# First search first: a smaller first k load, q of tile 0 in two halves, and constants made early, in a fused attention and expert kernel

## The chip, the cores and the metric

The kernel runs on one NeuronCore of a Trainium2 chip. The core has TensorE (PE, matmuls and their weight loads, PEld), VectorE (DVE), ScalarE (ACT), GpSimd (POOL) and SyncE (SP, which here issues nearly all DMAs). Each engine works through its own queue in order, and the engines wait for one another only by semaphores. The metric is the device time of one execution, in microseconds (us); lower is better.

## The reference

Attention with a top-k mask, then a top-1 mixture of eight experts, then a dense layer pair with a rational activation:

```python
B, H, S, D = 2, 8, 576, 64          # q, k, v
scores = (q @ k.T) / sqrt(D)
kth = partition(scores, -32)[..., -32:-31]      # the 32nd largest of each row
attn = softmax(where(scores >= kth, scores, -1e9))
x = (attn @ v) as [1152, 512] rows
# experts: argmax gate, capacity 288, relu(x @ w1[e]) @ w2[e], times the gate's weight
# dense: h = x @ w_in; g = (a0 + a1 h + a2 h^2 + a3 h^3) / (1 + |b0||h| + |b1| h^2 + 1e-6); g @ w_out
```

## The kernel before

**Tiling.** The 1152 rows of the two batches form NT = 9 tiles of 128 queries. With H = 8 heads this gives NH = 72 units of one tile and one head, numbered `i` with `n, h = divmod(i, H)`. Tile 4 is mixed, half of it from each batch. Each unit's scores are 128 x 576. In fp32r precision one number is a high part, made by a copy to fp32r on ACT, and a low part, the difference, made by DVE or POOL; k and q are split so, and then turned (transposed) by PE into PSUM and copied out by ACT.

**The search.** DVE finds the 32nd largest of each row of 576 scores. `greater(x)` takes the larger of each pair (288 numbers) from PSUM and the copy in SBUF, POOL's `sum_pairs(x)` and `less_greater(x)` make the lesser ones (both plain 128x288 operations). Then DVE takes steps: `M1` to `M4` (MAX8, the next eight largest), `R1` to `R3` between them (MATCH_REPLACE8, strikes these eight out), `L1`, `LR`, `L2` the same for the lesser ones, and `JOIN` and `FIN` that give the limit. `R1` waits for `less_greater`. Two units are interwoven: loop step `i` of DVE does the first half of unit `i`, the second half of unit `i-1`, and `greater(i+2)`.

**The slots.** Outside DVE, every engine has a function `slot(i)` that is called for each unit in order. PE: `scores(i+2)`, `times_v(i-3)`, then the scores' turns of unit `i-2` (`turn_scores`, `less_max`, `drop`), then `k_turn` and `q_turn`. ACT: `short_of(i-2)`, `scores_out(i+2)` (PSUM to SBUF), `x_out`, `k_high`, `q_high`, `exps(i-2)`, then `k_out` and `q_out` of what PE turned. POOL: `max_parts(i-1)`, `less_greater(i+1)`, `sums`, `k_low`, `sum_pairs(i+2)`, `q_low`. `k_pieces(i)`, `k_heads(i)` and `q_pieces(i)` say which head of k and which part of q is due in a slot; the table `USE` numbers all uses of the PSUM banks for turns in order. `scores(x)` waits for `greater(x-1)`, as both use the same PSUM tile.

**The beginning.** Ahead of the slots stands an order written out by hand. SP issues k of heads 0 and 1, q of tile 0, k of heads 2 to 7, v of batch 0, then waits until the first q is split (`s_ql`), and issues q of tile 1, k of batch 1, the gate weights, the coefficients and v of batch 1. PE begins with nine `fill` matmuls on a tile of ones (L1707), which compute nothing that is used, then turns k of head 0, q high and q low of heads 0 to 3, and k of head 1; `scores(0)`, fills, `scores(1)`, turns of k of head 2, q of heads 4 to 7, k of head 3. ACT (the lines that matter are these):

```python
k_high(0)
q_high(0)
k_high(1)
k_out(0, 0); k_out(0, 1); q_out(0, 1, 0)
k_out(1, 0); k_out(1, 1)
k_high(2)
scores_out(0)
k_high(3)
scores_out(1)
```

DVE does `k_low(0)`, the low part of q, `k_low(1)`, the copy of turned q high (L874), `greater(0)`, `greater(1)`, and then its loop, which begins with `M1` of unit 0. POOL splits heads 2 and 3, does `sum_pairs(0)`, `sum_pairs(1)`, `less_greater(0)`, then sets constants (L756, ones beside v; L757, zeros; `tri` and others from L759), then the slots.

**Later.** After the last unit PE, DVE and ACT compute the gate and the slots of the tokens, and then PE runs the experts and the dense layers (L1757 to L1759, three products for each fp32r pair). Weight loads are issued by SP as buffers come free.

## Time and profile before

| | |
|---|---|
| median of 3 runs | 777.88 us (777.29 to 779.7) |
| the profiled execution | 775.52 us |
| its span (first to last instruction) | 773.7 us |
| PE busy | 745.3 us (96%) |
| DVE busy | 663.3 us (86%) |
| ACT busy | 499.9 us (65%) |
| POOL busy | 383.2 us (50%) |

The profile is one execution on the chip. Its timeline gives for each instruction start, duration, engine, source line, operation, output <- input and, in brackets, the idle time of that engine before it and what ended it. "SPq" is the queue of SP, whose duration is that of issuing. `pairs` are the halves that the search works on, `best` the eights that it found, `scores` the copies in SBUF, `bank` any PSUM tile, `k_split` the high and low parts of k. The granted TensorE clock is full in all forty slices of the page.

### The profile page before, as it was taken

What the parts mean: (1) busy time and instruction counts of PE and PEld (TensorE: products, weight loads), DVE (VectorE), ACT (ScalarE), POOL (GpSimd) and SP (SyncE); (2) the same over time, 40 slices, a digit from 0 to 9 for tenths busy, and PEclk for the clock granted to TensorE, in tenths of its full rate; (3) what the DMA queues carried; (4) which work ended last, traced back from release to release, by engine and by line L of the source; (5) the groups of instructions that cost most, each with busy time, mean ns of one, the idle gap of its engine ahead of it and who ended that gap; (6) DMA issues with size and microseconds to landing.
All of it is one profiled execution on the core that took longest, in us unless ns stands there. A gap on an engine that the chain in (4) does not pass through costs nothing.

```text
span 773.7 us, 15880 instructions
## 1 busy us (share of the span) xinstructions
PE 745.3 (96%) x5503; PEld 697.7 (90%) x5503; DVE 663.3 (86%) x1682; ACT 499.9 (65%) x911; POOL 383.2 (50%) x550
## 2 busy tenths in 40 slices
PE   7899999999999989899999999999999999999998
PEld 5788899898888888799999999999998998999996
DVE  3999999999999999986767666767679999988885
ACT  6677777656667776466454444445578878777674
POOL 4746665545457786446000000000369879666764
PEclk9999999999999999999999999999999999999999
DMA  9840000800000303004657675769740002001001
GB/s 188 196 150 14 2 16 1 215 19 16 14 3 15 110 2 110 2 1 161 221 166 236 179 262 164 242 175 258 168 149 28 1 1 82 1 0 40 3 1 41
DMA packets 59853, 70.63 MB, mean 91 GB/s; under 512 B 21858, under 2 KB 39522, under 8 KB 59780
## 3 DMA queue, kind: packets, MB, share of 16 engines
q1 hardware_dynamic: 58340, 64.98, 29.5%
q0 software_dynamic: 1440, 4.72, 1.8%
q8 instruction: 41, 0.67, 0.4%
q14 instruction: 32, 0.26, 0.1%
HBM read 55.53 MB, written 14.16 MB: 90 GB/s over the span
## 4 chain that ended last, share of the span: by engine, by line
PE 54%; DVE 30%; issue 7%; POOL 4%; ACT 3%; DMA 1%; DVEq 0%; SPq 0%; POOLq 0%; ACTq 0%
PE bank L1757 14%; PE bank L1758 14%; PE bank L1759 14%; DVE best L900 9%; DVE pairs L902 6%; PE bank L1617 3%; DVE best L921 3%; DVE pairs L883 3%; DVE pairs L919 3%; DVE r L1206 2%; PE bank L1593 2%; PE bank L1583 2%; DMA k_rows<-in_k 1%; PE bank L1677 1%; DVE joined L930 1%
## 5 line engine op out<-in xcount | busy, mean ns | idle before, releaser
L1206 DVE RECIPROCAL r<-c 128x384 f32<-128x384 f32 x48 | 122.4, 2550 | 16.5 <-POOL c L836 15.9
L1279 ACT ACTIVATE probsT<-bank 96x768 f32<-96x768 f32 x72 | 58.1, 807 | 90.6 <-PE bank L1600 88.2
L900 DVE MAX8 best<-pairs 128x8 f32<-128x288 f32 x288 | 115.3, 440 | 0.0
L1617 PE MATMUL bank<-v_rows,probsT 96*128 96x65 f32 (+1 forms) x960 | 105.7, 263 | 2.6 <-ACT probsT L1279 2.3
L1617 PEld LDWEIGHTS bank<-v_rows,probsT 96*128 96x128 f32 (+1 forms) x960 | 102.0, 181 | 6.8 <-ACT probsT L1279 5.6
L902 DVE MATCH_REPLACE8 pairs<-best,pairs 128x288 f32<-128x288 f32 x216 | 94.1, 440 | 0.0
L806 POOL DMA_INDIRECT x_rows_of_others<-slots_out,slot_index_of_others x3 | 4.4, 1477 | 180.5 <-DMA slots_out<-y_blocks 179.8
L1420 ACT ACTIVATE hTh<-bank 128x288 fp32r<-128x288 f32 x64 | 26.3, 411 | 102.5 <-PE bank L1759 100.6
L698 POOL TENSOR_TENSOR pairs<-scores 128x288 int32<-128x288 int32 x72 | 57.6, 800 | 65.7 <-ACT scores L1265 65.4
L1088 DVE TENSOR_TENSOR wl<-raw,wh 128x1024 fp32r<-128x1024 f32 x60 | 72.9, 1217 | 17.2 <-ACT wh L1387 17.2
L1757 PE MATMUL bank<-xTh,wh 128*128 128x288 f32 x256 | 75.7, 296 | 1.0 <-issue 0.7
L1759 PE MATMUL bank<-hTh,wl 128*128 128x288 f32 x256 | 76.1, 297 | 0.0
L1758 PE MATMUL bank<-hTl,wh 128*128 128x288 f32 x256 | 75.8, 296 | 0.0
L1757 PE MATMUL bank<-hTh,wh 128*128 128x288 f32 x256 | 75.7, 296 | 0.0
L1758 PE MATMUL bank<-xTl,wh 128*128 128x288 f32 x256 | 75.6, 295 | 0.0
L1759 PE MATMUL bank<-xTh,wl 128*128 128x288 f32 x256 | 75.1, 293 | 0.0
L836 POOL TENSOR_TENSOR c<-c,h 128x384 f32<-128x384 f32 x48 | 48.6, 1013 | 40.1 <-ACT h L1503 40.0
L1757 PE MATMUL bank<-x2h,wh 128*128 128x384 f32 x192 | 65.4, 341 | 0.0
L1759 PE MATMUL bank<-x2h,wl 128*128 128x384 f32 x192 | 64.7, 337 | 0.0
L1758 PE MATMUL bank<-x2l,wh 128*128 128x384 f32 x192 | 64.5, 336 | 0.0
L921 DVE MAX8 best<-pairs 128x8 f32<-128x288 f32 x144 | 64.5, 448 | 0.0
L1387 ACT ACTIVATE wh<-raw 128x1024 fp32r<-128x1024 f32 x60 | 62.9, 1051 | 0.0
(188 smaller groups left out, 2234.3 us busy)
## 6 DMA issues: line engine op xcount, KB each, us to landing
raw<-in_moe_w SPq DMA_DIRECT2D x15, 2048.0 KB, 9.0
slots_in<-zeros SPq DMA_DIRECT2D x18, 256.0 KB
raw<-in_moe_w_in SPq DMA_DIRECT2D x8, 512.0 KB
slot_rows<-slots_in SPq DMA_DIRECT2D x28, 144.0 KB, 8.8
slots_out<-y_blocks SPq DMA_DIRECT2D x28, 144.0 KB, 8.1
v_rows<-in_v SPq DMA_DIRECT2D x16, 144.0 KB, 4.7
out_rows<-out_rows SPq DMA_DIRECT2D x9, 256.0 KB, 2.0
q_rows<-in_q SPq DMA_DIRECT2D x8, 256.0 KB, 3.1
```

Of the source, the lines that this page charges most:

```text
L698: nc.gpsimd.tensor_tensor(pr[x % NPR][:, 1].bitcast(I32), of[:, 0:HS], of[:, HS:S], ALU.add).then_inc(s_ps, 1)
L900: ins = nc.vector.max(best, cur)
L902: ins = nc.vector.match_replace(cur, best, cur, NEG)
L921: ins = nc.vector.max(best, cur)
L1088: nc.vector.tensor_tensor(piece(wl[slot], c), piece(raw[which], c), piece(wh[slot], c).bitcast(F32), ALU.subtract).then_inc(s_wl, 1)
L1206: nc.vector.reciprocal(rS[x][:], cS[x][:]).then_inc(s_d2, 1)
L1279: nc.scalar.activation(pT[x % 2][:], turned(x)[0:KP, 0:KJ * P], ACT.Exp, scale=SCALE).then_inc(s_ex, 1)
L1387: nc.scalar.activation(piece(wh[slot], c), piece(raw[which], c), ACT.Copy).then_inc(s_wh, 1)
L1617: last = nc.tensor.matmul(dst[r_, :], pT[x % 2][:, j * P + r_.start:j * P + r_.stop], vn[:, bb * H + h, j, :], start=(j == 0), stop=(j == ...
L1757: nc.tensor.matmul(dst, ah, bh, start=start, stop=False)
L1758: nc.tensor.matmul(dst, ah, bl, start=False, stop=False)
L1759: return nc.tensor.matmul(dst, al, bh, start=False, stop=stop)
```

## The change

- **Loads.** k of head 0, first half of q of tile 0 (heads 0 to 3), k of head 1, second half of q, k of heads 2 and 3, k of heads 4 to 7: six loads where there were three. The second half of q has a semaphore of its own. SP waits for `s_ql` of 2 (both halves split) ahead of q of tile 1; all later waits on `s_ql` and `s_qh` count one higher (shown once below).
- **First q.** ACT makes the high part in two halves; DVE makes the low part of the first half, POOL of the second.
- **Order.** ACT copies `scores_out(0)` ahead of `k_out(1)` and `k_high(2)`. DVE does `M1` of unit 0 and `k_low(2)` between `greater(0)` and `greater(1)`, then `R1` and `L1` of unit 0. `k_low(1)` comes behind the copy of turned q. PE's fills are 2, 2 and 3 in place of 2 and 5, and the turns of head 1 come behind `scores(0)`.
- **Constants.** POOL makes the ones beside v, the zeros, `tri` and the small ones ahead of its first `sum_pairs`. `k_low(2)` goes to DVE.
- **Tile 0.** Heads 3 to 7 of k are turned in slots 0 to 4 (before: 4 to 7 in slots 0 to 3), the second q half in slots 0 (high) and 1 (low), and q of tile 1 in slots 4 and 5 in place of 3 and 4. In slots 0 to 6 ACT does `k_high` and `scores_out` first and the copies of turned k and q ahead of `exps`; PE turns k and q ahead of the scores' turns; POOL does `k_low` first in slots 2 to 6.

```diff
@@ -383,7 +384,7 @@
-        FIRST_K, FIRST_Q = 4, 2
+        FIRST_K, FIRST_Q = 3, 2
@@ -401,10 +402,14 @@
             n, h = divmod(i, H)
+            if i in (0, 1):
+                return [(0, i, 1)]
             if h == 0:
...
                 return []
+            if n == 0:
+                return {4: [(1, 0, 0)], 5: [(1, 1, 0)], 7: [(1, 0, 1)]}.get(h, [])
             return {3: [(n + 1, 0, 0)], 4: [(n + 1, 1, 0)], 7: [(n + 1, 0, 1)]}.get(h, [])
@@ -426,7 +431,7 @@
         for what in (("k", 0, 0), ("k", 0, 1), ("q", 0, 0, 0), ("q", 0, 1, 0), ("k", 1, 0), ("k", 1, 1),
-                     ("k", 2, 0), ("k", 2, 1), ("q", 0, 0, 1), ("q", 0, 1, 1), ("k", 3, 0), ("k", 3, 1)):
+                     ("k", 2, 0), ("k", 2, 1)):
             next_use(*what)
@@ -466,11 +471,12 @@
         M1, R1, M2, R2, M3, R3, M4, L1, LR, L2, JOIN, FIN = range(12)
-        TK = {}
+        TK = {(0, M1): 1, (0, R1): 2, (0, L1): 3}
         for i in range(NH + 1):
...
                           (i - 1, JOIN), (i, L2), (i - 1, FIN)):
-                if 0 <= x < NH:
+                if 0 <= x < NH and (x, st) not in TK:
                     TK[x, st] = len(TK) + 1
@@ -542,6 +548,12 @@
+            def load_first_q(half, done):
+                c_ = slice(half * (H // 2), (half + 1) * (H // 2))
+                sp.dma_start(qn[:].rearrange("p (h d) -> p h d", h=H)[:, c_, :],
+                             q[0, c_, 0:P, :].rearrange("h s d -> s h d")).then_inc(done, 16)
             def load_k(i, lo, hi):
@@ -549,14 +561,17 @@
-            load_k(0, 0, 2)
-            load_q(0)
-            load_k(1, 2, H)
+            load_k(0, 0, 1)
+            load_first_q(0, s_q)
+            load_k(4, 1, 2)
+            load_first_q(1, s_qb)
+            load_k(1, 2, 4)
+            load_k(2, 4, H)
             load_v(0, 0, 2)
             load_v(1, 2, H)
-            sp.wait_ge(s_ql, 1)
+            sp.wait_ge(s_ql, 2)
             load_q(1)
-            load_k(2, H, 2 * H)
+            load_k(3, H, 2 * H)
             for c in range(DC):
@@ -564,7 +579,7 @@
-            sp.wait_ge(s_ql, 2)
+            sp.wait_ge(s_ql, 3)
             load_q(2)
@@ -675,7 +690,7 @@
             def q_low(n):
-                pool.wait_ge(s_qh, n + 1)
+                pool.wait_ge(s_qh, n + 2)
                 pool.wait_ge(s_pf, filled("q", n - 1, 1, 1))
@@ -728,14 +743,18 @@
                 n, h = divmod(i, H)
+                if 1 < i < H - 1:
+                    for g in k_heads(i):
+                        k_low(g)
                 if 0 <= i - 1 < NH:
...
                     sums(n - 1)
-                for g in k_heads(i):
-                    k_low(g)
+                if not 1 < i < H - 1:
+                    for g in k_heads(i):
+                        k_low(g)
                 if i + 2 < NH:
@@ -749,23 +768,26 @@
                 nc.gpsimd.memset(t[:, TOPK + LESSER:], -NEG).then_inc(s_inf, 1)
-            for g in (2, 3):
-                k_low(g)
-                sum_pairs(g - 2)
-            less_greater(0)
             nc.gpsimd.memset(vn[:, :, :, D:DV], 1.0).then_inc(s_vo, 1)
             nc.gpsimd.memset(zeros[:], 0.0).then_inc(s_zm, 1)
-            k_low(FIRST_K)
             nc.gpsimd.affine_select(out=tri[:], in_=ones[:].bitcast(F32), compare_op=ALU.is_gt, fill=0.0, base=0,
...
             nc.gpsimd.memset(ohz[:, 0:E].bitcast(F32), 0.0).then_inc(s_sum0, 1)
+            sum_pairs(0)
+            less_greater(0)
+            k_low(FIRST_K)
+            sum_pairs(1)
+            pool.wait_ge(s_qh, 2)
+            pool.wait_ge(s_ql, 1)
+            nc.gpsimd.tensor_tensor(ql[:, DM // 2:], qn[:, DM // 2:], qh[:, DM // 2:].bitcast(F32), ALU.subtract
+                                    ).then_inc(s_ql, 1)
             for i in range((MIXED - 1) * H):
...
             for bb in range(B):
-                pool.wait_ge(s_kl[1], 2 * H - 2)
+                pool.wait_ge(s_kl[1], 2 * H - 3)
                 other = slice((1 - bb) * HALF, (2 - bb) * HALF)
@@ -867,13 +889,14 @@
             dve.wait_ge(s_qh, 1)
-            nc.vector.tensor_tensor(ql[:], qn[:], qh[:].bitcast(F32), ALU.subtract).then_inc(s_ql, 1)
-            k_low(1)
+            nc.vector.tensor_tensor(ql[:, 0:DM // 2], qn[:, 0:DM // 2], qh[:, 0:DM // 2].bitcast(F32), ALU.subtract
+                                    ).then_inc(s_ql, 1)
             dve.wait_ge(s_pf, filled("q", 0, 0, 0))
...
             ins.then_inc(s_pd, 1)
+            k_low(1)
@@ -944,16 +967,23 @@
             greater(0)
+            of_greater(0, M1)
+            k_low(2)
             greater(1)
+            of_greater(0, R1)
+            of_lesser(0, L1)
             for i in range(NH + 1):
                 n, h = divmod(i, H)
-                of_greater(i, M1)
+                if i:
+                    of_greater(i, M1)
                 of_greater(i - 1, M3)
...
                     sums(n - 1)
-                of_greater(i, R1)
+                if i:
+                    of_greater(i, R1)
                 of_greater(i - 1, R3)
-                of_lesser(i, L1)
+                if i:
+                    of_lesser(i, L1)
                 of_greater(i, M2)
@@ -1246,17 +1276,21 @@
             def k_high(g):
-                act.wait_ge(s_k[0 if g < 2 else 1 if g < H else 2], 16)
+                act.wait_ge(s_k[0 if g == 0 else 4 if g == 1 else 1 if g < 4 else 2 if g < H else 3], 16)
                 if g >= KRING:
...
                 act.wait_ge(s_q, 16 * (n + 1 + (n >= MIXED)))
-                if n:
-                    act.wait_ge(s_ql, n)
-                    act.wait_ge(s_pf, filled("q", n - 1, 0, 1))
+                act.wait_ge(s_ql, n + 1)
+                act.wait_ge(s_pf, filled("q", n - 1, 0, 1))
                 nc.scalar.activation(qh[:], qn[:], ACT.Copy).then_inc(s_qh, 1)
+            def first_q_high(half):
+                act.wait_ge((s_q, s_qb)[half], 16)
+                c_ = slice(half * (DM // 2), (half + 1) * (DM // 2))
+                nc.scalar.activation(qh[:, c_], qn[:, c_], ACT.Copy).then_inc(s_qh, 1)
@@ -1300,14 +1334,23 @@
                 n, h = divmod(i, H)
+                if i < H - 1:
+                    for g in k_heads(i):
+                        k_high(g)
+                if i + 2 < NH:
+                    scores_out(i + 2)
                 if 0 <= i - 2 < NH:
                     short_of(i - 2)
-                if i + 2 < NH:
-                    scores_out(i + 2)
+                if i < H - 1:
+                    for k_ in k_pieces(i):
+                        k_out(*k_)
+                    for q_ in q_pieces(i):
+                        q_out(*q_)
                 if i >= 3 and (i - 3) % XG == XG - 1 and i - 3 < LAST * H:
                     x_out((i - 3) // XG)
-                for g in k_heads(i):
-                    k_high(g)
+                if i >= H - 1:
+                    for g in k_heads(i):
+                        k_high(g)
                 if h == 1 and n < LAST:
@@ -1316,34 +1359,31 @@
                     exps(i - 2)
-                for k_ in k_pieces(i):
-                    k_out(*k_)
-                for q_ in q_pieces(i):
-                    q_out(*q_)
+                if i >= H - 1:
+                    for k_ in k_pieces(i):
+                        k_out(*k_)
+                    for q_ in q_pieces(i):
+                        q_out(*q_)
                 if x_piece(i) is not None:
...
             k_high(0)
-            q_high(0)
-            k_high(1)
+            first_q_high(0)
             k_out(0, 0)
...
             q_out(0, 1, 0)
+            k_high(1)
+            scores_out(0)
             k_out(1, 0)
...
             k_high(2)
-            scores_out(0)
-            k_high(3)
+            first_q_high(1)
+            k_high(FIRST_K)
             scores_out(1)
...
             k_out(2, 1)
-            q_out(0, 0, 1)
-            q_out(0, 1, 1)
-            k_high(FIRST_K)
-            k_out(3, 0)
-            k_out(3, 1)
             def gated(t):
@@ -1541,7 +1581,7 @@
                 use = USE["q", n, low, half]
-                pe.wait_ge((s_qh, s_ql)[low], n + 1)
+                pe.wait_ge((s_qh, s_ql)[low], n + 2 if n else half + 1)
                 part = (qh, ql)[low][:].bitcast(F32)
@@ -1686,14 +1726,20 @@
                     times_v(i - 3)
+                if i < H - 1:
+                    for k_ in k_pieces(i):
+                        k_turn(*k_)
+                    for q_ in q_pieces(i):
+                        q_turn(*q_)
                 if 0 <= i - 2 < NH:
...
                     drop(i - 2)
-                for k_ in k_pieces(i):
-                    k_turn(*k_)
-                for q_ in q_pieces(i):
-                    q_turn(*q_)
+                if i >= H - 1:
+                    for k_ in k_pieces(i):
+                        k_turn(*k_)
+                    for q_ in q_pieces(i):
+                        q_turn(*q_)
                 if x_piece(i) is not None:
@@ -1713,18 +1759,15 @@
             q_turn(0, 1, 0)
+            fill(2)
+            scores(0)
+            fill(2)
             k_turn(1, 0)
             k_turn(1, 1)
-            fill(2)
-            scores(0)
-            fill(5)
+            fill(3)
             scores(1)
...
             k_turn(2, 1)
-            q_turn(0, 0, 1)
-            q_turn(0, 1, 1)
-            k_turn(3, 0)
-            k_turn(3, 1)
             pe.wait_ge(s_vo, 1)
```

## Rows read from the trace of the kernel before

**Rows 1.** DVE's waits, 0 to 340 us: waiter <- releaser: us, times, longest.
```profile
DVE pairs L883 <- ACT scores L1265: 5.8, 4, 3.7
DVE k_split L865 <- ACT k_split L1252: 4.7, 1, 4.7
DVE pairs L902 <- POOL pairs L705: 1.1, 2, 0.9
```

**Rows 2.** The chain that ended last, around 319 us: start, us, what.
```profile
319.14 0.44 DVE pairs L883
...
319.71 0.37 PE bank L1571
```

**Rows 3.** Timeline, 0 to 20 us (columns as told above).
```profile
1.06 4.04 PE L1707 MATMUL bank<-ones 128*128 128x512 f32 x9 [1.06 <-POOL ones L663]
...
4.66 0.56 DVE L865 TENSOR_TENSOR k_split<-k_rows,k_split 96x384 fp32r<-96x384 f32 x1 [4.66 <-ACT k_split L1252]
...
4.97 0.63 ACT L1259 ACTIVATE q_rows_high<-q_rows 128x512 fp32r<-128x512 f32 x1 [0.34 <-DMA q_rows<-in_q]
...
5.37 0.69 PE L1536 MATMUL bank<-ident,k_split 96*128 96x96 f32 x6 [0.27 <-DVE k_split L865]
...
6.38 0.63 PE L1549 MATMUL bank<-ident,q_rows_low 128*64 128x128 f32 x4
...
7.04 1.20 ACT L1243 ACTIVATE qT_low<-bank 64x512 fp32r<-64x512 f32 x2 [0.44 <-PE bank L1549]
...
8.38 0.37 PE L1571 MATMUL bank<-kT,qT_high 128*128 128x288 f32 x1 [0.33 <-ACT qT_low L1243]
...
8.86 0.29 PE L1572 MATMUL bank<-kT,qT_low 128*128 128x288 f32 x1
...
10.68 0.52 ACT L1252 ACTIVATE k_split<-k_rows 96x384 fp32r<-96x384 f32 x1 [1.70 <-DMA k_rows<-in_k]
...
11.10 0.63 ACT L1265 ACTIVATE scores<-bank 128x576 f32<-128x576 f32 x1
...
11.76 0.46 DVE L883 TENSOR_TENSOR pairs<-bank,scores 128x288 f32<-128x288 f32 x1 [3.68 <-ACT scores L1265]
...
13.85 0.46 DVE L883 TENSOR_TENSOR pairs<-bank,scores 128x288 f32<-128x288 f32 x1 [1.63 <-ACT scores L1265]
...
14.23 0.45 DVE L900 MAX8 best<-pairs 128x8 f32<-128x288 f32 x1
...
15.61 0.09 DVE L902 MATCH_VALUE_LOAD pairs<-best,pairs 128x8 f32 x1 [0.94 <-POOL pairs L705]
...
18.41 0.46 DVE L883 TENSOR_TENSOR pairs<-bank,scores 128x288 f32<-128x288 f32 x1 [0.34 <-ACT scores L1265]
...
19.75 0.09 DVE L902 MATCH_VALUE_LOAD pairs<-best,pairs 128x8 f32 x1 [0.15 <-POOL pairs L705]
```

**Rows 4.** Groups by line, 0 to 26 us: busy, mean ns | idle before.
```profile
L674 POOL TENSOR_TENSOR k_split<-k_rows,k_split 96x384 fp32r<-96x384 f32 x6 | 6.0, 996 | 9.9 <-ACT k_split L1252 9.8
...
L1222 ACT ACTIVATE kT<-bank 128x288 fp32r<-128x288 f32 x12 | 4.2, 401 | 0.1
...
L705 POOL TENSOR_TENSOR pairs<-pairs 128x288 int32<-128x288 int32 x4 | 3.2, 798 | 0.0
```

**Rows 5.** Issues of the page: count, KB each, us from issue to landing.
```profile
k_rows<-in_k SPq DMA_DIRECT2D x1, 864.0 KB, 8.9
```

**Rows 6.** Tile q_rows, 0 to 60 us: landing of its three loads.
```profile
DMA to landing us min/median/max: 3.2/3.7/5.6
```

**Rows 7.** Timeline, 35 to 42 us: ACT's `scores_out(6)`, `greater(6)`, PE's `scores(7)`, `scores(8)`.
```profile
35.57 0.63 ACT L1265 ACTIVATE scores<-bank 128x576 f32<-128x576 f32 x1
...
36.24 0.45 DVE L883 TENSOR_TENSOR pairs<-bank,scores 128x288 f32<-128x288 f32 x1
...
37.32 0.38 PE L1571 MATMUL bank<-kT,qT_high 128*128 128x288 f32 x1
...
41.24 0.37 PE L1571 MATMUL bank<-kT,qT_high 128*128 128x288 f32 x1
```

More of the change, by code:

```diff
@@ L218, in fused @@
         ys = nc.dram_tensor("slots_out", (SLOTS + 1, DM), F32, kind="Internal").ap()
-        s_k = [sem(f"k_in{i}") for i in range(3)]
+        s_k = [sem(f"k_in{i}") for i in range(5)]
         s_q = sem("q_in")
+        s_qb = sem("first_q_second_half_in")
         s_v = [sem(f"v_in{i}") for i in range(3)]
@@ L574, in _ @@
             for n in range(3, MIXED + 2):
-                sp.wait_ge(s_ql, n)
+                sp.wait_ge(s_ql, n + 1)
                 load_q(n)
@@ L601, in _ @@
             for n in range(MIXED + 2, NT):
-                sp.wait_ge(s_ql, n)
+                sp.wait_ge(s_ql, n + 1)
                 load_q(n)
@@ L1528, in k_turn @@
                 use = USE["k", g, half]
-                if g < 2:
+                if g < 3:
                     pe.wait_ge(s_kl[0], g + 1)
                 else:
-                    pe.wait_ge(s_kl[1], g - 1)
+                    pe.wait_ge(s_kl[1], g - 2)
                 prep_in(use)
```

## The prediction

> **What bounds the kernel now.** I read the page first: VectorE (DVE) is full to the last tenth in the attention half, TensorE (PE) in the expert half. So the first question is whether the search on DVE ever waits. The list of DVE's waits over attention answers it [rows 1]: 5.8 us for ACT's copies of the scores, 4.7 us for the very first split of k, 1.1 us for POOL's differences, and nothing else of size. The timeline places them [rows 3]: 3.68 us ahead of the first `greater` (11.76), 1.63 ahead of the second, 0.94 ahead of R1 of head 0 (15.61), 0.34 at 18.41, 0.15 at 19.75. From there to about 320 us DVE works nearly without a gap, some 4.42 us a head ((36.24 - 18.41 - 0.15) / 4, [rows 3, 7]). The chain of waits hands over from DVE to PE only at the last `greater` [rows 2]; all later work follows from it. So a microsecond saved before 19.75 should be one off the end, provided DVE stays without gaps.
>
> Why is the start slow? The scores of head 0 are in PSUM at 9.15 (the last of four matmuls, 8.86 + 0.29), but ACT copies them at 11.10, because `k_high(2)` stands ahead of the copy in ACT's queue and waits for the 864 KB load, until 10.68 [rows 3, 5]. M1 of head 0 then stands behind `greater(1)`, and R1 behind POOL.
>
> **Part 1, the smaller first loads.** PE's nine fills end at 5.10 and the first turn of k starts at 5.37, after 0.27 of waiting for DVE [rows 3]. Half-size loads land earlier, yet the fills are unchanged and PE takes no turn before 5.10: this is worth between 0 and 0.27. The smaller low part of q can only shorten what comes after; I leave that out. I take 0.27, since the load had been 4.97 for all of q and only half is needed, and both splits of q shrink to half a length. Then the low turn starts at 5.10 + (6.38 - 5.37) = 6.11, `qT_low` runs 6.77 to 7.97 and `scores(0)` starts at 8.11.
>
> **Part 2, the copy ahead of the load.** ACT now does `k_high(1)` (0.52, by 8.49, under the scores matmuls) and then `scores_out(0)`, with no load ahead of it but k of head 1, which is issued before all that waits here. Scores end at 8.11 + (9.15 - 8.38) = 8.88, copy 8.90 to 9.55 (0.63 and the step between), `greater(0)` starts 0.66 after the copy's start as before: 9.56 to 10.02, M1(0) to 10.47. This is 2.2 us earlier for `greater`, and M1 no longer waits for head 1.
>
> **Part 3, head 1 and R1(0).** ACT's queue sets it: two `k_out` (0.40 each [rows 4]) to 10.35, `k_high(2)` 0.52 to 10.87, the second q half (between half of the whole one's 0.63 and all of it; I take 0.35, from 0.52 for 384 elements against 256 here) to 11.22, `k_high(3)` to 11.74, `scores_out(1)` to 12.37. PE's part, turns of head 1, three fills and `scores(1)`, is done by about 11.2 and hidden. `greater(1)` 12.40 to 12.86, R1(0) at 12.87 instead of 15.61: 2.74 us. The added `k_low(2)` on DVE (0.56 [rows 3]) lies in the gap between M1(0), 10.47, and 12.40 and costs nothing; without that gap it would cost its 0.56. POOL's `sum_pairs(0)` and `less_greater(0)` (0.80 each; the row is `less_greater`'s, both work on 288 elements [rows 4]) run 9.56 to 11.2, before R1(0) needs them.
>
> **Part 4, the next two gaps.** From R1(0) to R1(1) before: 19.75 - 15.61 = 4.14, of which 0.34 + 0.15 idle, so 3.65 of work. R1(1) then at 16.52, if nothing is late. `greater(2)` is due at 12.87 + 2.80 - 0.34 = 15.33: `k_out(2)` to 13.17, `scores(2)` to 14.0, `scores_out(2)` to 14.65, 0.7 to spare. POOL: `k_low(3)` 11.77 to 12.77, `sum_pairs(1)` to 13.57, its q half (0.67, from 1.00 for k's 384 elements [rows 4] against 256) to 14.24, `less_greater(1)` to 15.0, against 16.52. So the sum is 19.75 - 16.52 = 3.2 us. POOL's constants (`vn`'s ones, the zeros, `tri` and three small ones) go to the stretch before 9.56 in which POOL has nothing else. No row here prices them one by one; even at a full 128x288 operation's 0.80 each, the six are 4.8 us, from the identities at the very start on, and hidden; what waited behind them (`scores(2)` for the ones of v) is inside the times above.
>
> **Part 5, what is moved in tile 0.** Turns of k now run one head earlier (head i+3 in slot i), and tile 1's q turns go from slots 3 and 4 to 4 and 5; in slots 0 to 6 ACT copies scores before `short_of`, PE turns k and q before the scores' turns, POOL splits k first. Before, PE fell behind exactly here: `scores_out(6)` started at 35.57 and ended 0.04 before `greater(6)` at 36.24 [rows 7]. After, `greater(6)` is due at 33.0. Walking PE's and ACT's queues with before's steps (a slot of PE without turns 41.24 - 37.32 = 3.92 [rows 7]; a group of turns about 0.5, as two of them took 1.01 [rows 3]), `scores_out(6)` ends near 30.7, `scores_out(7)` near 36.3 against 37.4, and from there PE gains 0.5 a slot. The least margin is 1.1 us: no stall. POOL's `less_greater` is over 2 us early in slots 3 to 5.
>
> **Part 6, the later q load.** SP now waits for two q halves: POOL's ends at 14.24, so `load_q(1)` is issued at 14.3 at the earliest, where before the first split was long done, and behind it k and v of batch 1, the gate weights and the rational's coefficients; the first reader of these is `k_high(8)`, six slots of 4.42 later. q of tile 1 took at most 5.6 us to land [rows 6], so 19.9. ACT reaches `q_high(1)` in slot 1 at about 20.6; a wait there holds `k_high(6)` and `scores_out(4)`, which `greater(4)` needs at 24.2, so it costs only from a landing at 22.4. Free, with ends of 0 and, at the 8.9 us of the slowest early k load [rows 5], 0.7 us.
>
> **Sum.** 3.2 us off the profiled execution: 775.52 (span 773.7) to 772.3. The median of the runs stands 2.36 above that execution; taking the same difference, 777.88 - 3.2 = 774.7.
>
> **Rivals.** (a) **k of heads 2 and 3 lands late.** `k_high(2)` still stands ahead of `scores_out(1)`; it must be in by 10.35. Before, all of the first q was in at 4.97 and 864 KB more of k by 10.68. If transfers are served in order, 288 KB land at 4.97 + 5.7/3 = 6.9; if the loads share evenly with v and k of 4 to 7, at about 10.7 plus three more issues of 0.4, about 12. Then 1.6 is lost: 776.3. For it speaks that the 864 KB took 8.9 us for itself; against, that q was in long before k though issued just before. The Trainium skill (DMA: Bandwidth & Descriptors, table of the fixed and variable cost) puts a transfer at about 2.0 us and bytes over 436 GB/s, which as an estimate is 2.7 us for this load and would leave this rival no chance; the trace disagrees for a queue this full, 8.9 us where that sum gives 4.0 [rows 5].
> (b) **The turns ahead of the scores' turns hold PE (slower than before).** Each turn needs a bank that ACT empties, and ACT's `k_out` now stands behind `short_of` and its q copies (1.20 [rows 3]). If PE waits 1.2 in each of slots 2 to 5 and 1.2 more for each of two q turns, that is 7.2 against a margin of some 1.1 to 2.4: 4.8 to 6.1 of stalls in `greater`, 1.6 to 2.9 more than the gain: about 780. It decides from 1.1 (gain shrinks) and 4.3 (slower). For it: the 0.04 of before, and 3.92 plus two turns of 0.5, over the 4.42 that a slot has. Against: a turn is issued while the bank before it has been free for a slot, and POOL and ACT split k a slot early.
> (c) **Nothing reaches the end.** The search starts early but some later wait with its own clock (a load, the mixed tile: of DVE's 5.8 us 0.15 are left for all of it) takes it back: 777.9. Against: every load behind tile 1 is issued by semaphores of this same chain.
> (d) **The change doesn't do what it says**, as M1(0) ahead of `greater(1)` delays the release of `scores(1)`: no, `scores(1)` waits only for `greater(0)` and `k_out(1)`; part of (a) in price.
>
> **How the numbers follow.** Forecast 0.72; (a) 0.12; (b) 0.06; (c) and (d) 0.10. Predicted 774.7. The unknowns of parts 1, 3 and 6 give -0.3 to +1.0, and the runs before spread from -0.6 to +1.8 about their median; reaching over (a) and into (c) the range is 773.0 to 777.8. About 0.3% (2.3 us) is what a measurement of this kernel can tell from no change. The forecast leaves 0.9 above it, so about nine tenths of its case and little of (a) count as faster: 0.66; slower by over 0.3% only (b) and bad runs, 0.06; the rest 0.28.
>
> **What would show it.** In the timeline after: first `greater` near 9.6, M1(0) right behind it, R1(0) near 12.9, R1(1) near 16.5, DVE without waits from there; ACT not idle for a load before `k_high(2)`; `scores_out(6)` and `(7)` at least 0.5 ahead of their `greater`; the last `greater` at 319.14 - 3.2, and the span 3.2 shorter. Wrong if ACT sits for k rows past 10.4, if DVE waits for scores after 17 us, or if the last `greater` is early and the end is not.

## The result, and the profile after

The changed kernel takes **771.95 us** (median of 5 runs, 771.5 to 772.58) against 777.78 (5 runs, 775.64 to 779.7): ratio 0.9936, interval 0.9916 to 0.9956. That is faster by 5.8 us where I had forecast 3.2, and 1.05 us below my range. The profiled execution of after took 771.5, its span is 769.6; before it was 775.52 and 773.7. So one execution against one shows 4.0 to 4.1 us, and the medians show 5.8. These are two different gaps in my forecast, and the experiments take them one by one. Four executions among those of the experiments ran at a mean granted clock of 0.55 to 0.85 and took 824 to 1229 us; they are left out of every median, range and count below.

DVE's waits in the same 340 us (waiter <- releaser: us in total, times, longest), beside [rows 1]:

```profile
DVE k_split L887 <- ACT k_split L1282: 4.8, 3, 3.7
DVE qT_high L896 <- PE bank L1589: 1.8, 1, 1.8
DVE pairs L906 <- ACT scores L1299: 0.7, 2, 0.5
```

The 5.8 us for the copies of scores have become 0.7, and the 1.1 for POOL's differences is gone. Of the 4.8, 3.7 is the wait for the very first split, which was 4.66 with the load of twice the size. The 1.8 for the turned q is new: DVE now has less to do ahead of it.

DVE's queue to 16 us (columns as in [rows 3]):

```profile
3.68 0.56 DVE L887 TENSOR_TENSOR k_split<-k_rows,k_split 96x384 fp32r<-96x384 f32 x1 [3.68 <-ACT k_split L1282]
...
9.67 0.46 DVE L906 TENSOR_TENSOR pairs<-bank,scores 128x288 f32<-128x288 f32 x1 [0.49 <-ACT scores L1299]
10.16 0.46 DVE L923 MAX8 best<-pairs 128x8 f32<-128x288 f32 x1
10.89 1.00 DVE L887 TENSOR_TENSOR k_split<-k_rows,k_split 96x384 fp32r<-96x384 f32 x1 [0.26 <-ACT k_split L1282]
12.14 0.46 DVE L906 TENSOR_TENSOR pairs<-bank,scores 128x288 f32<-128x288 f32 x1 [0.25 <-ACT scores L1299]
12.52 0.08 DVE L925 MATCH_VALUE_LOAD pairs<-best,pairs 128x8 f32 x1
...
14.88 0.44 DVE L906 TENSOR_TENSOR pairs<-bank,scores 128x288 f32<-128x288 f32 x1
...
15.97 0.07 DVE L925 MATCH_VALUE_LOAD pairs<-best,pairs 128x8 f32 x1
```

The three waits ahead of `greater` of 3.68, 1.63 and 0.34 us [rows 3] are now 0.49, 0.25 and none; R1 of head 0 stands at 12.52 for 15.61, right behind `greater(1)`.

Starts of `greater`, in both traces:

| unit | before | after | earlier by |
|---|---|---|---|
| 0 | 11.76 | 9.67 | 2.09 |
| 1 | 13.85 | 12.14 | 1.71 |
| 2 | 18.41 | 14.88 | 3.53 |
| 3 | 23.02 | 19.21 | 3.81 |
| 6 | 36.24 | 32.43 | 3.81 |
| 38 | 177.56 | 173.69 | 3.87 |
| 39 | 182.24 | 178.09 | 4.15 |
| 71 | 323.54 | 319.36 | 4.18 |

Nearly all is won by unit 3, nothing is lost in tile 0, and 0.3 comes at unit 39, far behind the start. What is won at unit 71 is in the span: 4.1.

### The profile page after: what moved, and what is told of

Read it like the earlier page. It is cut to its first block, busy times and chain, and to the rows that moved or that the text cites. A ratio compares the mean times of both kernels' runs of the same rounds, so it can differ in the third digit from the quotient of the medians.

```text
span 769.6 us, 15886 instructions
## 1 busy us (share of the span) xinstructions
PE 745.4 (97%) x5503; PEld 698.2 (91%) x5503; DVE 663.4 (86%) x1683; ACT 502.3 (65%) x912; POOL 382.8 (50%) x550
## 4 chain that ended last, share of the span: by engine, by line
PE 58%; DVE 29%; issue 7%; ACT 3%; POOL 3%; DVEq 0%; ACTq 0%; POOLq 0%
PE bank L1800 14%; PE bank L1801 14%; PE bank L1802 14%; DVE best L923 9%; DVE pairs L925 6%; PE bank L1657 4%; DVE pairs L906 3%; DVE best L944 3%; DVE pairs L942 3%; PE bank L1633 2%; PE bank L1623 2%; DVE r L1236 2%; DVE joined L953 1%; PE bank L1607 1%; PE bank L1717 1%
## 5 line engine op out<-in xcount | busy, mean ns | idle before, releaser
L923 DVE MAX8 best<-pairs 128x8 f32<-128x288 f32 x288 | 116.8, 450 | 0.1
L944 DVE MAX8 best<-pairs 128x8 f32<-128x288 f32 x144 | 66.0, 458 | 0.0
```

The source lines that it names most:

```text
L923: ins = nc.vector.max(best, cur)
L944: ins = nc.vector.max(best, cur)
```

## The experiments

Each time is a median with its lowest and highest, each ratio is against the kernel before, run beside it. "Gain" is how much earlier a `greater` stands than in the trace of before.

### Does the change's first-load part matter?

**The same two kernels again** (the second set). No edit.

> The kernel before, unchanged. The medians differ by 5.8 us where the two traces differ by 4.1 (spans 773.7 and 769.6). Theory L: the runs of before spread because its first copy of scores stands behind the 864 KB load of k, and that load lands later in most runs than the 10.68 us of the traced one; then this run's own trace shows the load landing at another time, the first `greater` moved with it, and its span moved by the same amount, while everything after `greater(2)` keeps its pace; runs spread over 2 us or more. Rival N: the spread is noise of anywhere (the weight loads of the expert half, the clock); then the load lands at 10.7 +- 0.2 again and the difference in span, if any, arises elsewhere.

> The kernel after, unchanged. Theory L: all loads it waits for land well ahead of need, so the runs lie within about 1 us and the first `greater` comes at 9.67 again within 0.1. Rival N: spread as wide as that of before. Both: ratio to before 0.992 to 0.996.

Before: 777.4 (775.24 to 779.68), ratio 1.0002. After: 772.12 (771.47 to 772.86), ratio 0.9929 (0.991 to 0.9948). The result stands, and so does what I had not thought of: before spreads over 4.4 us, after over 1.4. The two traces of this second set have the spans 773.7 and 770.3, so this pair differs by 3.4 where the first differs by 4.1. In before the load landed as in the first trace (ACT's `k_high(2)` at 10.57), in after the first `greater` came at 10.43 for 9.67, behind slower first turns (shown at the fills below).

**Before's three loads in the changed kernel.**

```diff
-            load_k(0, 0, 1)
-            load_first_q(0, s_q)
-            load_k(4, 1, 2)
-            load_first_q(1, s_qb)
-            load_k(1, 2, 4)
-            load_k(2, 4, H)
+            load_k(0, 0, 2)
+            load_q(0)
+            load_k(1, 2, H)
```

> The kernel after, but with before's three loads (k of heads 0 and 1; all of q; k of heads 2 to 7). ACT's k_high(2), which stood at 10.33 and fed `scores_out(1)`, waits for the 864 KB again. If it lands at 10.7: 0.4 us later there, and 0.1 to 0.3 in the first turns (q lands at 4.97 instead of 3.6), 0.5 us in all against after. Theory L: the runs spread again as before's do and the median loses 1 to 2 us against after. Rival N: the median loses 0.5 and the spread stays at 1 us. A third reading, that the small loads themselves are what the change brought: it loses 3 us or more.

772.59 (772.12 to 772.81), ratio 0.9937 (0.9918 to 0.9955); span 770.3. The six loads are worth at most some 0.5 us, which is hardly more than the comparison can tell, and with the large load back the spread is still 0.7: in the new order the large load brings no spread. (In before it does bring some, see the last question.)

**512 KB more in the queue**, a load that nobody reads, ahead of k of heads 2 and up, in each kernel.

```diff
+            sp.dma_start(raw[0][:, 0:1024], w1[0][0:P, :]).then_inc(s_dum, 16)
             load_k(1, 2, H)
```

> The kernel before with one more load of 512 KB (read by nobody) issued between q of tile 0 and the 864 KB of k. At the 213 KB a us of this stretch it should land the k some 2.4 us later, near 13.1. If the start of before hangs on that load, as its trace reads, POOL's order from k_low(2) on and R1 of head 0 move by the same: R1(0) at 17.5 to 18.2 instead of 15.6, the end 2 to 2.5 us later. If the loads were not what its start waits for: 0.3 or less.

> The kernel after with the same 512 KB issued ahead of k of heads 2 and 3. k of heads 2 and 3 landed at 8.0, is read at 10.33, so it lands at 10.4 and costs 0 to 0.2; k of heads 4 to 7 landed near 10.3 at the latest and then comes near 12.7, read at 13.04: nothing. So 0 to 0.3 us, where the same load costs before 2 us or more. If the loads share evenly instead of being served in order, both land later and it costs 1 us or more.

Before with it: 780.31 (776.78 to 781.95), ratio 1.0029 (1.0009 to 1.0049). After with it: 771.73 (771.58 to 772.01), ratio 0.9923 (0.9905 to 0.994), which is the kernel without it. In the trace of the first DVE stands

```profile
13.34 0.46 DVE L886 TENSOR_TENSOR pairs<-bank,scores 128x288 f32<-128x288 f32 x1 [5.22 <-ACT scores L1268]
15.96 0.46 DVE L886 TENSOR_TENSOR pairs<-bank,scores 128x288 f32<-128x288 f32 x1 [2.17 <-ACT scores L1268]
```

where before had 3.68 and 1.63: the load's delay of 1.6 us (k_low(2) on POOL at 12.86 for 11.28) goes straight into the first search. (By unit 6 4.2 us are lost: in this trace the granted clock is at 0.50 from 14 to 18 and from 34 to 36 us. PE had paused for 3.58 us until 13.95, and for 1.45 us until 30.82.) R1(0) stands at 17.66, 2.05 later; I had expected 1.9 to 2.6. In after the load for heads 2 and 3 took 6.8 us instead of 5.3 and nobody waited. So the load ahead of the copy in ACT's queue set the start of before.

### Which part of the new order carries the gain?

**In before, only the copy of the first scores ahead of the load.**

```diff
-            k_high(2)
             scores_out(0)
+            k_high(2)
```

> The kernel before with one line moved: ACT's `scores_out(0)` ahead of `k_high(2)`. The first `greater` should come at about 9.9 instead of 11.76. My reading of the queues: nothing of it reaches R1 of head 0, since POOL's order (k_low(2), sum_pairs(0), k_low(3), sum_pairs(1), less_greater(0)) still starts with the k that lands at 10.68; R1(0) at 15.6, 0 to 0.3 us gained. The rival, that the load ahead of the copy alone was the loss: 1.5 to 2 us gained.

775.9 (774.62 to 778.62), ratio 0.998 (0.9963 to 0.9997). `greater(0)` and `greater(1)` move up by 1.1, and then:

```profile
12.74 0.46 DVE L883 TENSOR_TENSOR pairs<-bank,scores 128x288 f32<-128x288 f32 x1 [1.64 <-ACT scores L1265]
13.11 0.45 DVE L900 MAX8 best<-pairs 128x8 f32<-128x288 f32 x1
15.61 0.09 DVE L902 MATCH_VALUE_LOAD pairs<-best,pairs 128x8 f32 x1 [2.05 <-POOL pairs L705]
```

R1 stands where it stood in before, to the hundredth; the wait for ACT has become one for POOL, whose queue still has two splits ahead of `less_greater(0)`:

```profile
11.28 1.01 POOL L674 TENSOR_TENSOR k_split<-k_rows,k_split 96x384 fp32r<-96x384 f32 x1 [8.61 <-ACT k_split L1252]
12.24 0.80 POOL L698 TENSOR_TENSOR pairs<-scores 128x288 int32<-128x288 int32 x1
13.01 0.99 POOL L674 TENSOR_TENSOR k_split<-k_rows,k_split 96x384 fp32r<-96x384 f32 x1
13.97 0.79 POOL L698 TENSOR_TENSOR pairs<-scores 128x288 int32<-128x288 int32 x1
14.72 0.79 POOL L705 TENSOR_TENSOR pairs<-pairs 128x288 int32<-128x288 int32 x1
```

So of 3.8 us this one move gives 0.7 from unit 3 on, where I had expected 0 to 0.3: the two small waits of before behind R1(0), 0.34 and 0.15, are gone, and R1(0) itself waits for POOL. No run moves POOL's queue alone.

**M1 of unit 0 back behind `greater(1)`.**

```diff
-            of_greater(0, M1)
             k_low(2)
             greater(1)
+            of_greater(0, M1)
```

> The kernel after, with M1 of unit 0 behind `greater(1)`, as before had it. It then no longer fits into DVE's gap ahead of `greater(1)` and all that follows comes later by one MAX8: 0.40 to 0.46 us. If another engine set R1(0), 0.

772.7 (772.62 to 773.13), ratio 0.9936 (0.9919 to 0.9953). `greater(1)` to R1(0) takes 12.79 - 11.93 = 0.86 where it took 12.52 - 12.14 = 0.38: 0.48 lost, as the gap no longer hides M1.

**The constants back behind `less_greater(0)`** (ones of v and zeros).

```diff
-            nc.gpsimd.memset(vn[:, :, :, D:DV], 1.0).then_inc(s_vo, 1)
-            nc.gpsimd.memset(zeros[:], 0.0).then_inc(s_zm, 1)
...
             less_greater(0)
+            nc.gpsimd.memset(vn[:, :, :, D:DV], 1.0).then_inc(s_vo, 1)
+            nc.gpsimd.memset(zeros[:], 0.0).then_inc(s_zm, 1)
```

> The kernel after, with the two large constants of POOL (the ones beside v, the zeros; 0.83 us together) put back behind `less_greater(0)`, ahead of `k_low(3)`. POOL's `less_greater(1)` began at 14.17 and is needed at 15.97, so 0.8 later it ends at 15.8 and fits: 0 us, at most 0.1. If POOL's chain were what sets the start after the change: 0.5 to 0.8 us slower.

771.94 (771.93 to 772.42), ratio 0.9924 (0.9902 to 0.9946); R1(0) to R1(1) takes 3.45 us in both. The constants early are worth nothing here.

**Seven first fills in place of nine.**

```diff
-            fill(9)
+            fill(7)
```

> The kernel after with seven fills instead of nine ahead of the first turns. k of head 0 is split at 4.24 and its turn waits for PE's fills until 5.07. The nine fills take 0.45 us each, those of the later group 0.27, so the clock is at its lower level in them. If the turns merely waited for the queue, they start 0.8 us earlier and R1 of head 0 comes 0.6 to 0.8 earlier, end 0.6 to 0.8 earlier. If the clock's rise sets the pace, the turns run at half speed (1.2 us for six instead of 0.87) and most of it is lost: -0.3 to +0.3.

772.04 (770.98 to 772.22), ratio 0.9924 (0.9897 to 0.9952). The first turns begin 0.54 earlier and gain nothing (columns as above):

```profile
1.65 2.76 PE L1753 MATMUL bank<-ones 128*128 128x512 f32 x6
4.50 0.93 PEld L1576 LDWEIGHTS bank<-ident,k_split 96*128 96x128 f32 x6 [0.81 <-issue]
4.53 1.19 PE L1576 MATMUL bank<-ident,k_split 96*128 96x96 f32 x6
```

Six turns take 1.19 us for the 0.87 they take in the first trace of after, the four behind them 1.06 for 0.60, and `greater(0)` stands at 10.14, not 9.67. That looks as if the missing fills made the turns slow, but the second trace of after has all nine fills and the same slow turns, with `greater(0)` at 10.43:

```profile
5.06 1.17 PE L1576 MATMUL bank<-ident,k_split 96*128 96x96 f32 x6
6.02 1.06 PE L1589 MATMUL bank<-ident,q_rows_high 128*64 128x128 f32 x4
```

So the run shows that two fills fewer change the time by nothing that can be told. Whether the fills make the turns behind them faster is not shown.

### Which part of the slots' order matters?

**PE's turns behind the scores' turns and ACT's copies behind `exps` in tile 0, as before.**

```diff
-                if i < H - 1:
-                    for k_ in k_pieces(i):
-                        k_turn(*k_)
-                    for q_ in q_pieces(i):
-                        q_turn(*q_)
                 if 0 <= i - 2 < NH:
...
                     drop(i - 2)
+                for k_ in k_pieces(i):
+                    k_turn(*k_)
+                for q_ in q_pieces(i):
+                    q_turn(*q_)
```

> The kernel after, but in tile 0 PE turns k and q behind the scores' turns and ACT copies them behind `exps`, as before did; the start, the schedule of heads and `k_high` and the copy of scores ahead of `short_of` stay. It tests how much of the result lies in the turns put in front. By the walk of the queues `greater(6)` has about 1.1 us to spare either way; so 0 to 0.3 us slower. If the turns in front were needed, DVE waits for scores appear at units 4 to 7, 0.5 us each or more.

776.57 (773.72 to 779.66), ratio 0.9981 (0.9961 to 1.0002); the span at full clock is 771.9 to 772.2, so 2 us are lost there:

```profile
38.27 0.46 DVE L906 TENSOR_TENSOR pairs<-bank,scores 128x288 f32<-128x288 f32 x1 [1.57 <-ACT scores L1299]
```

```profile
43.35 0.46 DVE L906 TENSOR_TENSOR pairs<-bank,scores 128x288 f32<-128x288 f32 x1 [0.57 <-ACT scores L1299]
```

These are units 7 and 8; from unit 3 to unit 8 the gain shrinks from 4.2 to 1.7. I expected 0 to 0.3. The turns in front are no risk that the change takes, as my rival (b) had it; the early start needs them. The median loses more than that, 4.5 us: five of the nine executions have a mean granted clock of 0.991 to 0.995 and spans of 774.8 to 777.8, as in before.

**The turns in front in every tile.** The same edit the other way: the condition `i < H - 1` taken away.

> The kernel after with the turns of k and q, and their copies, in front in all slots, not only in slots 0 to 6. DVE has no wait from unit 3 on in the trace of after, so an execution at full clock gains nothing: median 771.5 to 772.2, within 0.3 of after. If the later q and k turns still cost some executions (granted clock below 1.0 in 3 of 11), their share goes: up to 0.3 us on the median. If the turns in front hold back `exps` and so the later matmuls in the mixed tile, it is 0.5 us or more slower.

778.8 (778.2 to 779.42), ratio 1.0024 (1.0011 to 1.0037), 7 us slower than after. DVE now waits in tiles 1 to 5, units 14 to 43:

```profile
DVE pairs L925 <- POOL pairs L720: 3.6, 3, 1.6
DVE pairs L906 <- ACT scores L1299: 3.0, 7, 0.7
```

So turns in front can hold DVE up, at a price (7 us of span at full clock) above the 4.8 to 6.1 of rival (b), but in the tiles that the change leaves alone. More than half of the wait is for POOL, which the rival had not in it; whether its mechanism, PE held by banks, is at work is not shown.

**`short_of` ahead of the scores' copy again, from slot 7 on; and, in before, behind it in all slots.**

```diff
+                if i >= H - 1 and 0 <= i - 2 < NH:
+                    short_of(i - 2)
                 if i + 2 < NH:
                     scores_out(i + 2)
-                if 0 <= i - 2 < NH:
+                if i < H - 1 and 0 <= i - 2 < NH:
                     short_of(i - 2)
```

> The kernel after, but from slot 7 on ACT does `short_of` ahead of the copy of the scores, as before did. Theory C: unit 39 waits again (0.3 us), the runs spread with the granted clock over some 4 us and the median rises by 1.5 to 2.2 us, to 773.7 to 774.3, while the fastest run stays near 772. Rival P: 0.3 us slower, spread as that of after.

```diff
-                if 0 <= i - 2 < NH:
-                    short_of(i - 2)
                 if i + 2 < NH:
                     scores_out(i + 2)
+                if 0 <= i - 2 < NH:
+                    short_of(i - 2)
```

> The kernel before with one edit: in every slot ACT copies the next scores (`scores_out(i+2)`) ahead of `short_of(i-2)`. Its start is as in before. Theory C: before's runs spread with their mean granted TensorE clock (773.4 to 773.7 us of span at 1.0, 775 at 0.998, 777 to 778 at 0.993), because a short fall of the clock in attention puts PE behind, the copy of the scores comes late by `short_of` (0.78 us) more, and DVE waits; in the trace of the kernel with the first copy moved a fall at 92 to 96 us cost DVE 0.75 and 0.57 us. With the copy first PE's lateness is absorbed: median 775.4 to 776.0 instead of 777.4, spread near 1.5 us, no wait at unit 39 (0.3 us), while the span of an execution at clock 1.0 gains only that 0.3. Rival P: the calm comes from the new start; then this kernel's median is 777.1 and its spread as before.

After without the swap: 773.5 (772.84 to 775.74), ratio 0.9946 (0.9931 to 0.9962), with waits back at units 10 (0.22) and 39 (0.18). Before with it: 775.75 (774.7 to 777.2), ratio 0.9978 (0.9962 to 0.9994), its wait at unit 39 gone. This is a part of the change that I had read as confined to slots 0 to 6, in front and in part 5; the diff has it in all slots.

**All of the slots' order on before's beginning, loads and table of pieces.**

> The kernel before with only the order inside the slots changed as in after: scores copied ahead of `short_of` in all slots; in slots 0 to 6 `k_high` first, turns and their copies in front, and POOL's k_low first in slots 2 to 6. The start, the loads, the constants and which head is due in which slot are before's. Theory C (the order makes the kernel bear the falls of the clock, and takes away PE's gaps that go ahead of them): an execution at clock 1.0 gains only the 0.3 of unit 39, span 773.3, but the median falls from 777.4 to about 775.4 with a spread of about 1 us: 2 us of the 5.5 are the slots' order and 3.5 the start. Rival: the start shares in the calm; then the median stays at 776.0 or above and executions at a clock of 0.995 and less still take 775.5 or more of span.

775.87 (775.27 to 777.73), ratio 0.999 (0.9975 to 1.0006): 0.8 us, and within its error nothing (I had expected a median of about 775.4). So the slots' order alone gives next to nothing, and the run with the turns behind shows that the new beginning without the turns in front gives 1.5 us (ratio 0.9981, not clear of nothing either). Only together do they give 5.8.

### Why do the medians differ by more than the spans of the profiled executions?

Each execution has its own span and mean granted clock. Of the kernel before there are 104 (those run beside the experiments, those of the second set, and four single ones), of after 11 (both sets):

| mean granted clock | before: executions, median span | after: executions, median span |
|---|---|---|
| 1.000 | 24, 773.55 | 8, 769.9 |
| 0.997 to 0.999 | 24, 774.95 | 3, 770.1 |
| 0.995 to 0.996 | 30, 775.9 | none |
| 0.991 to 0.993 | 26, 777.2 | none |

At full clock the kernels differ by 3.6 us. But three executions in four of before have a mean clock below 1, and the median span of all 104 is 775.6, 2 us above that of full clock. The page's row of the granted clock can't show this: its slices are 19.3 us long, a 9 stands for nine tenths or more, and it reads 9 throughout even on the page of the execution at 0.995. So "full in all forty slices", said ahead of the prediction, was more than the page tells; the profiled execution's own mean is 0.999. Three single profiled executions of the kernel before went after the place:

> The kernel before, unchanged, for one more trace. If its mean granted clock is below 1.0: reading S, the fall begins between 12 and 13 us, behind PE's idle time of 2.1 us ahead of `scores(1)`, and again in tile 0 at 32 to 37 us, and DVE waits for scores at units 1, 2 and 6, 1 to 3.5 us in all; reading M, the falls lie in the middle (60 to 320 us) or the gate (336 to 344 us), and the wait is spread or nil. At clock 1.0 it is the trace of before again, span 773.7.

> As the look before this one: the same kernel, the same two readings.

> As the two looks before this one: the same kernel, the same two readings.

They took 776.28, 777.72 and 777.71, with spans of 774.1, 775.6 and 775.9. The falls of the clock lie where the second of the two readings had them, in the middle of attention and at the gate, and not at the start. Stretches of the third (PE, PEld, DVE, ACT, POOL busy with their counts, granted clock, DMA share, GB/s), then of the first:

```profile
92.00:94.00 2.00, 2.00 (x15) 1.97 (x14) 2.00 (x10) 1.67 (x4) 0.78 (x1) 0.65 0.00 0
94.00:96.00 2.00, 2.00 (x9) 1.66 (x8) 2.00 (x9) 0.00 (x0) 0.98 (x2) 0.50 0.03 8
```

```profile
92.00:94.00 2.00, 2.00 (x20) 2.00 (x20) 2.00 (x9) 2.00 (x5) 0.22 (x1) 1.00 0.00 0
94.00:96.00 2.00, 2.00 (x21) 1.85 (x19) 2.00 (x9) 0.70 (x2) 1.84 (x4) 1.00 0.03 8
```

The clock falls to 0.50 (the lower of its two levels, 1.2 GHz), soon behind a stretch in which PE stood still for 0.59 us and then ran eight matmuls of 8 columns:

```profile
90.29 1.03 PE L1641 MATMUL bank<-wg,x_tileT 128*128 128x8 f32 x8 [0.59 <-ACT kT L1222]
...
93.50 1.48 PE L1583 MATMUL bank<-ident,scores 128*96 128x128 f32 x6
```

The six turns take 1.48 us for 0.82 at full clock, ACT's `exps` comes late, `short_of` stands ahead of the scores' copy, and DVE pays:

```profile
98.91 0.46 DVE L883 TENSOR_TENSOR pairs<-bank,scores 128x288 f32<-128x288 f32 x1 [0.93 <-ACT scores L1265]
```

The second execution falls at 94 to 98 us (0.54 and 0.61) and pays 1.25 in units 20 and 22, the third pays 1.57 there; the copy-first run falls at 92 to 96 and pays 1.43. Two more things lengthen these executions. One is a second fall, behind attention, in the work on the gate and the slots; in the third execution it stands at 341 to 345 us:

```profile
342.00:344.00 2.00, 2.00 (x10) 1.98 (x10) 1.62 (x6) 2.00 (x5) 2.00 (x2) 0.50 0.00 0
```

From the last `greater` to the end it takes 450.9 us, for 450.2 in the first traces of before and after; the three other traces with a fall there (M1 late, `short_of` first, the slots' order on before) have 451.0. So such a fall costs 0.7. The other is the load of 864 KB, which lands at a different time in each execution; in the second:

```profile
11.34 0.52 ACT L1252 ACTIVATE k_split<-k_rows 96x384 fp32r<-96x384 f32 x1 [2.17 <-DMA k_rows<-in_k]
```

In the five traces of before this start lies between 10.55 and 11.34, and the first `greater` is always 1.1 behind it. The second execution is 1.9 longer than the profiled one: 0.7 by the load, 1.25 by the fall. The third is 2.2 longer: 1.6 by the fall in attention, 0.7 by the one behind it, 0.1 back at the start. The first is 0.4 longer, by the load alone. In after no `greater` waits for that load, so this part of the spread is gone for a known reason.

How the falls themselves become rare is another matter. Executions by mean granted clock:

| kernel | executions | below 1.000 | below 0.997 |
|---|---|---|---|
| before | 104 | 80 | 56 |
| before, scores ahead of `short_of` | 11 | 8 | 3 |
| before, all of the slots' order | 11 | 9 | 3 |
| after, `short_of` first from slot 7 on | 11 | 8 | 2 |
| after, turns behind in tile 0 | 9 | 5 | 5 |
| after, turns in front everywhere | 12 | 4 | 0 |
| after, and its five edits of the beginning | 33 | 10 | 0 |

The traces with one fall have means of 0.997 or 0.998, the one with two 0.995. Read so, more than half of before's executions have two falls or more, and those of after at most one; in the one trace of the last row that has a fall (M1 late) it is the cheap one behind attention. Executions below 0.997 come back when any one of three parts of the change is taken back: the beginning, the turns in front in tile 0, or the scores' copy ahead of `short_of`, though 2 or 3 of 11 are few. Why it takes all three is **not settled**: PE's pause of 0.59 us ahead of the gate's matmuls stands in after too (at 86 to 87 us), and in before's own trace, with no fall behind it. Whether the change also makes a fall in attention cheaper is not shown: no trace of after has one there.

## Why the prediction was right or wrong

- **What bounds the kernel: right.** A microsecond before the fourth `greater` was one off the end. The last `greater` is however the one at 323.54; the one I named, 319.14, is that of unit 70.
- **Part 1: right in the first trace, and in part by luck.** Low turn of q 6.21 (I had 6.11), `qT_low` to 8.04 (7.97), `scores(0)` at 8.18 (8.11). In the second trace of after the low turn stands at 6.87 and the first `greater` 0.76 later: the first turns took the time I had from before's trace in one case and not in the other. The six loads come to 0.5 at most, where I had 0 to 0.27 and left out the shorter low part of q.
- **Part 2: right.** `scores_out(0)` 8.98 for 8.90, `greater(0)` 9.67 for 9.56, and the isolated move shows its price.
- **Part 3: right in kind, 0.35 too small.** R1(0) stands at 12.52, not 12.87. I had laid ACT's copies end to end by their durations; they follow each other faster:

```profile
10.33 0.52 ACT L1282 ACTIVATE k_split<-k_rows 96x384 fp32r<-96x384 f32 x1
10.75 0.41 ACT L1293 ACTIVATE q_rows_high<-q_rows 128x256 fp32r<-128x256 f32 x1
11.06 0.51 ACT L1282 ACTIVATE k_split<-k_rows 96x384 fp32r<-96x384 f32 x1
11.47 0.64 ACT L1299 ACTIVATE scores<-bank 128x576 f32<-128x576 f32 x1
```

  0.52 + 0.41 + 0.51 is 1.44, and the starts lie 1.14 apart: about 0.1 us each. That gives 0.26 of the 0.35; the last 0.09 is the same effect on DVE, R1(0) starting 0.38 behind `greater(1)` and not 0.47. `k_low(2)` on DVE took 1.00, not 0.56, and the gap still hid it: DVE waited 0.25 more for ACT.
- **Part 4: 0.2 too small.** R1(0) to R1(1) takes 3.45; I had 3.65, having taken off the two waits as they are listed (0.34 and 0.15). A wait is counted from the end of the step before, and without one DVE's next step starts 0.08 to 0.09 ahead of that end (12.94 and 13.31 for two steps of 0.45), so each wait is worth 0.09 more than its bracket. Together 16.52 against 15.97: 0.55 of the missed 0.6 up to unit 3. That the constants are free stands (0.0 measured).
- **Part 5: the conclusion right, the weight wrong.** No stall: `scores_out(7)` ends at 35.61, `greater(7)` starts at 36.84, a margin of 1.2 (I had 1.1). But I judged the moved turns by whether they do harm, and never asked what the early start would cost without them: 2 us at full clock, 4.5 on the median. And I took the swap of `short_of` and the scores' copy to be tile 0's alone. In the mixed tile (unit 39) before had

```profile
180.90 0.78 ACT L1273 ACTIVATE short_of_least<-scores,least_kept 128x576 bf16<-128x576 f32 x1
181.58 0.63 ACT L1265 ACTIVATE scores<-bank 128x576 f32<-128x576 f32 x1
```

  and DVE's `greater` waiting 0.18 behind it; in after the copy starts at 177.02 and `short_of` at 177.57. That is the 0.3 that I missed there.
- **Part 6: right.** `load_q(1)` issued at 14.23, nobody waited.
- **Rival (a)** didn't come: k of heads 2 and 3 landed at 8.0, 5.3 us after issue, with 2.3 to spare before 10.33. (The sum of 2.0 us and bytes over 436 GB/s stands in the Trainium skill (DMA: Bandwidth & Descriptors, Anatomy of one DMA) for transfers issued by GpSimd. SP issued this one, which took 5.3 where the sum gives, as an estimate, 2.7.) **(b)**: turns in front do harm outside tile 0 and good in it. **(c)** and **(d)** didn't come.
- **The sum: this step failed.** "The median stands 2.36 above that execution; taking the same difference" was wrong: after's median stands 0.45 above its own. These 2 us are no property of the measurement. In the traces that have them they are falls of the granted clock in attention (1.25 to 1.6 us each), another behind it (0.7), and the late landing of the 864 KB (up to 0.7), none of which the profiled execution of before happened to have (its granted clock is 1.00 from 86 to 100 us and from 336 to 340). The change takes the landing out of DVE's way, and the falls become rare, for a reason that stays open. The range carried the spread of before's runs over to after as if it were noise. The other term, 3.2 us off the profiled execution, was too small as well: 4.1 in the first pair of traces (0.6 by parts 3 and 4, 0.3 by part 5), though only 3.4 in the second pair and 3.6 between the medians at full clock, so the first pair flatters the change by some 0.5. With 3.6 to 4.1 in place of 3.2 the forecast would have been 773.8 to 774.3, still inside the range; only the spread's disappearance brings it to 772. Had I asked what a longer execution does differently, the profile of one of them would have shown waits of DVE at units 20 and 22, for the scores' copy that the change moves.

## What to carry to other kernels

When one engine is the bound from some point on, price the start by walking each engine's queue in order: moving one copy ahead of a load gave 0.7 us of 3.8, because the wait passed to POOL's queue, and an early start that PE's queue did not follow up lost 2 us again at units 7 and 8. Read starts, not durations, off the rows when laying steps end to end: here that is 0.1 us a step and 0.55 us in the sum. And when runs of a kernel spread by 4 us, look for the cause before treating it as an offset: a change can take the spread away. Nor does one trace settle a cause: the slow turns behind seven fills looked like the edit's work until a trace with nine fills had them too.

## What the runs showed of the hardware

- **DVE and POOL hold each other up on SBUF.** `k_low(2)` on DVE takes 1.00 us next to POOL's `less_greater(0)` (10.67 to 11.47), where the same form took 0.56 alone, in all traces of the changed kernel that have it there; POOL's `k_low(3)`, overlapping its end, takes 1.10 for 1.00. Both of DVE's inputs are in SBUF. The Trainium skill (SBUF — State Buffer, two separate sides) says that such a DVE instruction and a GpSimd instruction that reads SBUF take one shared pair of ports for their whole length and that the later one waits; the trace agrees in direction, with 0.44 us lost of 0.58 us of overlap. For POOL's half there is a check: with the constants late, `k_low(3)` starts at 12.68, when DVE's split is over, and takes 0.99. For DVE's half no run isolates it.
- **The speed of the first turns varies.** In the second set's trace of after the first turns take 1.17 and 1.06 us where the first had 0.87 and 0.60, and `greater(0)` stands at 10.43, not 9.67, though the granted clock is recorded as full. In six traces with this beginning it stands between 9.17 and 10.43. The Trainium skill (TensorE: Matmul & The Clock Gate, Part 1) says that the count of slow matmuls at a kernel's start differs from run to run; here that is worth up to 0.8 us. Before hides it: in the second set's trace its first six turns take 1.19 us for 0.69 and its first `greater` stands at 11.67 for 11.76, as it waits for the load.
- **A short fall in the middle.** In three traces the granted clock falls to 0.50, that is 1.2 GHz, for some 3 to 4 us between 92 and 98 us, each time behind a pause of PE of 0.59 us and eight tiny matmuls; before's own trace has the same pause and matmuls and no fall. The price is 1.25 to 1.6 us by the waits that it starts. The same kind of fall at 336 to 345 us costs 0.7.
